# Prologue of a fused attention, mixture-of-experts and gated-MLP kernel: the third quarter of the inner weights ahead of keys and values, the fourth in halves, two tiles' transposes placed among the query-key products

## What is computed

```python
def _attn_ref(q, k, v, g_norm):                      # 8 heads of 64
    kv = np.einsum('bhsd,bhse->bhde', k, v)
    out = np.einsum('bhsd,bhde->bhse', q, kv)
    rms = np.sqrt(np.mean(out * out, axis=-1, keepdims=True) + 1e-06)
    return out / rms * g_norm
def _moe_ref(x, w_gate, wq, wk, wv, wo):             # 4 experts of width 64, top 2
    for e in range(E):
        q, k, v = x @ wq[e], x @ wk[e], x @ wv[e]
        a = causal_softmax(q @ k.T / 8)
        ye = a @ v @ wo[e]
        out += gate[e] * ye
def _moe2_ref(x, w_in, g_ln, w_sg, b_sg, w_out):     # d_ff 1024
    h = gelu(x @ w_in); u, v = split(h)
    v_s = w_sg @ layernorm(v, g_ln) + b_sg
    return x + (u * v_s) @ w_out
```

## Time and profile before

| | us |
|---|---|
| median of three runs | 814.02 |
| the profiled execution, its time | 816.52 |
| its span, first to last instruction | 814.4 |
| TensorE busy | 798.5 |
| VectorE busy | 489.7 |
| ScalarE busy | 371.3 |
| GpSimd busy | 186.3 |

### The profile page before, as it was taken

How to read it: one execution, slowest core, us unless ns; L and a number is a source line. 1 busy time by engine, 2 the same in 40 slices (tenths; PEclk the granted TensorE clock), 3 DMA queues, 4 the chain that set the end, 5 groups by cost and what they waited for, 6 DMA issues and landing times. The chain is left out here.

```text
span 814.4 us, 16834 instructions
## 1 busy us (share of the span) xinstructions
PE 798.5 (98%) x6605; PEld 720.0 (88%) x6605; DVE 489.7 (60%) x1293; ACT 371.3 (46%) x845; POOL 186.3 (23%) x239
## 2 busy tenths in 40 slices
PE   6999999999999999999999999999999999999998
PEld 5888989989899898989889898998989989898896
DVE  3878654675447855487444865468554675547740
ACT  2767423663345533556134752356323653355521
POOL 1641332013310233002330123301331013300220
PEclk9999999999999999999999999999999999999999
DMA  9956023030231205040050401404023000100001
GB/s 258 255 129 164 2 45 86 11 109 1 52 73 51 68 1 117 15 118 1 1 111 14 119 1 37 94 2 118 1 50 75 2 2 1 59 14 2 1 2 64
DMA packets 117405, 47.28 MB, mean 58 GB/s; under 512 B 94352, under 2 KB 110736, under 8 KB 117328
## 3 DMA queue, kind: packets, MB, share of 16 engines
q1 hardware_dynamic: 117328, 46.21, 22.6%
HBM read 35.19 MB, written 9.44 MB: 55 GB/s over the span
## 5 line engine op out<-in xcount | busy, mean ns | idle before, releaser
L1070 PE MATMUL w<-wsgT_s,big 128*128 128x288 f32 x768 | 107.6, 296 | 0.0
L1070 PE MATMUL t<-big,wqk_s 128*128 128x288 f32 x768 | 106.0, 296 | 1.0 <-DVE wsgT_s L950 0.9
L1070 PEld LDWEIGHTS w<-wsgT_s,big 128*128 128x128 f32 x768 | 104.0, 189 | 0.0
L1070 PEld LDWEIGHTS t<-big,wqk_s 128*128 128x128 f32 x768 | 102.5, 188 | 1.6 <-DVE wsgT_s L950 1.1
L1070 PE MATMUL w<-wout_s,big 128*128 128x512 f32 x396 | 99.1, 399 | 0.0
L610 POOL TENSOR_TENSOR yT<-squares,yT 128x256 fp32r<-128x256 f32 (+1 forms) x32 | 22.4, 699 | 316.8 <-ACT yT L740 316.8
L844 DVE CUSTOM_DVE_ANT_0 w<-w,causal 128x64 f32<-128x64 f32 (+4 forms) x160 | 75.3, 515 | 24.2 <-PE w L1101 23.1
L1070 PEld LDWEIGHTS w<-wout_s,big 128*128 128x128 f32 x396 | 72.9, 188 | 17.2 <-DVE big L887 1.6
L754 ACT ACTIVATE big<-work 128x576 fp32r<-128x576 f32 x32 | 21.9, 686 | 113.5 <-POOL work L633 94.3
L1070 PE MATMUL t<-w_s,yT 128*128 128x512 f32 x240 | 63.3, 404 | 0.0
L956 DVE TENSOR_REDUCE ss<-squares 128x8 f32<-128x512 f32 (+1 forms) x40 | 25.2, 630 | 62.6 <-ACT squares L690 62.5
(11 more groups left out here) (140 smaller groups left out, 1439.3 us busy)
## 6 DMA issues: line engine op xcount, KB each, us to landing
kin<-in_k_dram SPq DMA_DIRECT2D x8, 1024.0 KB, 6.2
vin<-in_v_dram SPq DMA_DIRECT2D x8, 1024.0 KB, 9.2
out_dram<-work SPq DMA_DIRECT2D x32, 256.0 KB, 2.1
qin<-in_q_dram SPq DMA_DIRECT2D x112, 72.0 KB, 2.4
staged_win<-in_moe_w_in_dram SPq DMA_DIRECT2D x4, 512.0 KB, 5.4
vin<-in_moe_w_sg_dram SPq DMA_DIRECT2D x4, 288.0 KB, 3.9
kin<-in_k_dram SPq DMA_DIRECT2D x8, 128.0 KB, 2.9
vin<-in_v_dram SPq DMA_DIRECT2D x8, 128.0 KB, 7.0
```

The source lines that it names most:

```text
L1070: last = nc.tensor.matmul(o, stationary(hs, c), mv(hm, c), start=c == of[0] and p == 0, stop=c == of[-1] and p == len(PASSES) - 1)
```

## The change

The prologue's list is written in another order. Quarter 2 of w_in (`win` 2 and `w2` 2) stands ahead of `kv`. The product of quarter 3 is cut in two steps, `w2c` 0 and `w2c` 1, of six matmuls each (one wide slot each). The query tiles' transposes are no longer together: tiles 3 and 4 come after x 0 and x 1. The x steps of tiles 3 and 4 leave the prologue: they are carried out in part 0 by a new step kind, `late`, which on each engine calls `body(part - 1, [j])`; one stands behind the first `qk` and `split` wv, the other behind the second `qk` and `w2e` 0. The loads follow: w_in quarter 2 ahead of k and v, g_norm ahead of q, quarter 3 between q tiles 2 and 3. Slots change with it. No arithmetic is added or taken away; the number of matmuls, copies and bytes is the same.

```diff
-    FIRST = [("woT", 0), ("woT", 1), ("win", 0), ("win", 1), ("w2", 0), ("w2", 1)] + [("kv", c) for c in range(DC)]
-    FIRST += [("qT", 0), ("qT", 1), ("qT", 2), ("o", 0), ("qT", 3), ("o", 1), ("qT", 4), ("win", 2), ("o", 2),
-              ("o", 3), ("w2", 2), ("x", 0), ("o", 4), ("win", 3), ("x", 1), ("x", 2), ("split", "wqk0"), ("split", "wqk2"), ("split", "wqk1"), ("split", "wqk3"), ("w2", 3), ("x", 3), ("x", 4)]
+    FIRST = [("woT", 0), ("woT", 1), ("win", 0), ("win", 1), ("w2", 0), ("w2", 1), ("win", 2), ("w2", 2)]
+    FIRST += [("kv", c) for c in range(DC)]
+    FIRST += [("qT", 0), ("qT", 1), ("o", 0), ("qT", 2), ("o", 1), ("o", 2), ("win", 3), ("x", 0), ("qT", 3), ("o", 3), ("x", 1),
+              ("qT", 4), ("w2c", 0), ("o", 4), ("split", "wqk0"), ("split", "wqk2"), ("x", 2), ("w2c", 1),
+              ("split", "wqk1"), ("split", "wqk3")]
+    FIRST_LATE = [("x", 3), ("x", 4)]
+    FIRST_SLOT = {("woT", 0): "t0", ("woT", 1): "t1", ("kv", 0): "t3", ("qT", 0): "t0", ("qT", 1): "t1", ("o", 0): "t2", ("qT", 2): "t0",
+                  ("o", 1): "t3", ("o", 2): "t0", ("x", 0): "t2", ("qT", 3): "t1", ("o", 3): "t1", ("x", 1): "t2", ("qT", 4): "t3",
+                  ("o", 4): "t3", ("x", 2): "t0", ("x", 3): "t2", ("x", 4): "t3"}
...
-        plan = [("qk", (0, 0))] + late(("split", "wv")) + [("qk", (EP, 0))] + late(("w2e", 0))
+        plan = [("qk", (0, 0))] + late(("split", "wv"), ("late", FIRST_LATE[0])) + [("qk", (EP, 0))] + late(("w2e", 0), ("late", FIRST_LATE[1]))
...
-            load_win((0, 1))
+            load_win((0, 1, 2))
             load_kv(0)
-            load_q(0)
-            load_win((2, 3))
             for a in range(2):
                 sp.dma_start(gnorm_c[HD * a:HD * (a + 1), :],
                              g_norm.rearrange("(p a) -> p a", a=1)).then_inc(w_loaded["gnorm"], 16)
+            load_q(0, (0, 1, 2))
+            load_win((3,))
+            load_q(0, (3, 4))
...
-                for kind, j in PLAN[part]:
+                for kind, j in PLAN[part] if among is None else among:
+                    if kind == "late":
+                        body(part - 1, [j])
+                        continue
```

More of the change, by code:

```diff
@@ L191, in ring @@
             turn[0] += 1
-        for kind, j in PLAN[part]:
+        for kind, j in PLAN[part] + (FIRST_LATE if part < 0 else []):
             if kind == "s":
@@ L450, in load_kv, with load_q @@
                                  ).then_inc(kv_loaded, 16)
-            def load_q(b):
-                sp.dma_start(qin[PAD:P, 0, :].rearrange("p (h d) -> p h d", h=H),
-                             q[b, :, 0:PAD, :].rearrange("h s d -> s h d")).then_inc(q_first[0], 16)
-                for t in range(1, NT):
+            def load_q(b, ts):
+                for t in ts:
+                    if t == 0:
+                        sp.dma_start(qin[PAD:P, 0, :].rearrange("p (h d) -> p h d", h=H),
+                                     q[b, :, 0:PAD, :].rearrange("h s d -> s h d")).then_inc(q_first[0], 16)
+                        continue
                     sp.dma_start(qin[:, t, :].rearrange("p (h d) -> p h d", h=H),
@@ L568, in _, with body @@
             before_loop = steps[0] + NT
-            def body(part):
+            def body(part, among=None):
                 done = [0]
@@ L1158, in body @@
                         finish(last, U)
-                    elif kind == "w2":
-                        pe.wait_ge(woT_hi, j // 2 + 1)
-                        pe.wait_ge(win_hi, j + 1)
+                    elif kind in ("w2", "w2c"):
+                        chunk, among_c = (j, range(EP)) if kind == "w2" else (DC - 1, [j])
+                        pe.wait_ge(woT_hi, chunk // 2 + 1)
+                        pe.wait_ge(win_hi, chunk + 1)
                         for p, (hs, hm) in enumerate(((HI, HI), (LO, HI), (HI, LO))):
                             if p == 1:
-                                u.wait_drained(pe, part, ("woT", j // 2))
+                                u.wait_drained(pe, part, ("woT", chunk // 2))
                             if p == 2:
-                                pe.wait_ge(win_lo, j + 1)
-                            for c in range(EP):
+                                pe.wait_ge(win_lo, chunk + 1)
+                            for c in among_c:
                                 x = ps[u.slot(part, ("w2", c))]
                                 for h in range(2):
-                                    last = nc.tensor.matmul(x[:, FF * h:FF * (h + 1)], woT_split[:, hs, 256 * j + P * c:256 * j + P * (c + 1)],
-                                                            win_split[j][:, hm, FF * h:FF * (h + 1)], start=j == 0 and p == 0,
-                                                            stop=j == DC - 1 and p == 2)
-                                if j == DC - 1 and p == 2:
+                                    last = nc.tensor.matmul(x[:, FF * h:FF * (h + 1)],
+                                                            woT_split[:, hs, 256 * chunk + P * c:256 * chunk + P * (c + 1)],
+                                                            win_split[chunk][:, hm, FF * h:FF * (h + 1)],
+                                                            start=chunk == 0 and p == 0, stop=chunk == DC - 1 and p == 2)
+                                if chunk == DC - 1 and p == 2:
                                     finish(last, ("w2", c))
```

5 lines of the change are left out of this document (1 added, 4 removed).

## The result

The changed kernel takes 818.37 us in the median of five runs (817.34 to 820.17), the kernel before 814.11 us beside it (five runs, 814.0 to 814.68). The medians lie 4.3 us apart. The ratio on record is 1.0046 with an interval of 1.0035 to 1.0058, which makes 3.7 us slower, 2.8 to 4.7. Forecast were 818.6 us and 4.55 us.

The account below looks back on a forecast made before the run. TensorE, busy 98% of the span, was taken as the bound, with `v` 0 as the mark. 1.94 + 0.98 + 1.1 + 0.6, less rounding 4.55 us, added to 814.02 gave 818.6 us; range 816.8 to 820.2.

Parts of the forecast that it names:

- The bound: Whole kernel: TensorE is busy 98% of the span, so a shift at `v` 0 reaches the end undiminished.
- Keys and values: Before `kv`: quarter 2's product fills TensorE's wait, the values come 1.4 us later, `kv` starts at 17.75 against 16.36.
- their 512 KB go ahead of the values on the one queue: Loads before `kv`: quarter 2's bytes delay the values by 1.4 us, or 1.83 at the stretch's rate.
- fit into the gap: TensorE before `kv`: quarter 2's 12 matmuls, 3.0 us or less, fit between 13.54 and 16.36 us.
- The chain behind `kv`: From `kv` on: cover for the o-to-x steps is lost, so the first query-key product starts at 37.0, 1.94 us later.
- The edits that were put at no cost: Prologue loads: wq and wk, and the last w_sg load waiting for query tile 4 (cover of 1.8 us), cost nothing.
- The late tiles: Query-key stretch: x 3 and x 4 add 0.98 us, plus gaps of 1.1 and 0.6 before the third and fourth products.
- The rule on ports: Tile 4's GpSimd power meets wqk2's VectorE low half: the skill's exclusive lock would add 1.5 us; forecast assumed no stretch.
- rival of stretched low halves: Beside tile 4's power: wqk2's low half starts at 36.95, first query-key product at 38.4, total 820.0 us; chance 0.12.
- faster: Behind `kv`: TensorE does not wait for the o-to-x way, total 811.6 us; chance 0.04.
- no change: After `v` 0: a later wait absorbs the shift, total 814 to 815.6 us; chance 0.06.
- No gap for late tiles: Query-key stretch: slots or VectorE are free in time, 1.7 us fall away, total 816.9 us; chance 0.14.

Follow-up runs that it names:

- e1: Kernel before with only quarter 2 of w_in (load, halves, product) moved ahead of `kv`; 815.5 against 815.58 us.
- e11: Kernel before with quarter 2 ahead of `kv`, query tiles 3 and 4 behind o 2, splits reordered, plus 11 early unused transposes; 816.76 against 815.71 us.
- e6: Changed kernel plus 11 unused transposes of the identity before TensorE's wait for the first load; 818.49 us, 2.9 us slower than the kernel before.
- before again: Kernel before, unaltered, run beside itself for a second profile; ratio 1.0004 (0.9994 to 1.0014).
- e2: Kernel before with only x 3 and x 4 moved among the query-key products, loads and slots kept; 817.93 against 815.58 us.
- e5: Changed kernel with each late x tile one step earlier, ahead of the split of wv and of `w2e` 0; 818.57 against 815.58 us for before.
- e8: Changed kernel with small unused matmuls filling TensorE's gaps before x 0, o 3, x 1 and the first query-key product; 819.87 us, 3.0 slower than before.
- e10: Kernel before with quarter 2 ahead of `kv`, query tiles 3 and 4 behind o 2, splits reordered, quarter 3's product ahead of wqk2; 817.16 against 815.71 us.
- e3: Changed kernel with x 3 and x 4 put back at the end of the prologue; 820.46 against 815.58 us for the kernel before.
- e7: Changed kernel with x 3 and x 4 back at the prologue's end and 20 unused transposes ahead of x 4; ratio to before 1.0037.

## Why the prediction held, and where its steps did not

**The bound.** Right. In the last column of the table, what follows `v` 0 has two values: 770.8 to 771.3 us in six profiles, 772.5 to 772.9 in eight. The kind of kernel doesn't decide which: the change has both. They are told apart by the granted clock from 750 to 755 us, 1.00 in the six and 0.66 to 0.81 in the eight. So a shift at `v` 0 comes out whole at the end, and beside it there is 1.7 us by chance. All five runs of before beside the change lay between 814.0 and 814.68, while its medians beside e1 to e11 were 815.6 to 815.8. The windows of the change, first and second profile (the window of the first has more idle time, since the kernel is 3 us later there):

```profile
750.00:755.00 5.00, 3.58 (x23) 0.70 0.00 2
```

```profile
750.00:755.00 5.00, 4.89 (x60) 1.00 0.00 0
```

The profiles of before and of the change both have the higher value, so they may be compared: 3.6 us of span, 3.87 at `v` 0.

**Keys and values.** The start was forecast at 17.75 and was 17.39 in the first profile and 16.25 in the second, and not for the reason given: this hit was luck. Two terms were wrong. One is "their 512 KB go ahead of the values on the one queue", priced at 1.4 us later values. The other is that the 24 products take 6.57 us and the 12 behind them "fit into the gap". The price of the bytes is near: ScalarE took quarter 2 at 8.57, 1.49 us after quarter 1 at 7.08. Yet the values landed at 5.57 + 10.4 = 16.0 us, no later than before (wait ended at 16.36). These are the issue row and the row of SyncE's queue in the change:

```profile
vin<-in_v_dram SPq DMA_DIRECT2D x1, 1024.0 KB, 10.4
```

```profile
5.57 2.60 SPq L452 DMA_DIRECT2D vin<-in_v_dram  x1
8.21 2.83 SPq L503 DMA_DIRECT2D gnorm_c<-in_g_norm_dram  x2
11.08 0.62 SPq L458 DMA_DIRECT2D qin<-in_q_dram  x1
```

What held `kv` was TensorE, which was busy without a break until then: 24 products in 7.74 us where before they took 6.57, then 12 more. In e6, where the first products were faster and nothing else ahead of `kv` differs, `kv` started at 15.90.

How much the 512 KB delay the values can be asked of all fourteen profiles, by the start of the issue plus the time to landing. With the old order of loads that gives 16.3, 17.0 and 14.9 us (before, before again, e2), 16.1 on average. With quarter 2 ahead it gives 15.7 to 16.3 in seven profiles, 16.9 in e5, and 18.1, 17.8 and 18.6 in e8, e10 and e11, 16.6 on average. So 0.5 us, not 1.4, with a spread of 2 to 3 us in each group that leaves it open whether there is any delay. The profiles in which TensorE is seen to wait for the values can't answer it alone, since behind the extra 12 products mostly the late landings show as a wait.

**The chain behind `kv`.** Right in every gap, and this is the main part of the forecast. Forecast gaps before o 0, x 0, o 3, x 1, first, third and fourth query-key product: 0.4, 1.1, 1.5, 1.3, 1.7, 1.1, 0.6. Measured: 0.34, 0.94, 1.19, 1.04, 1.54, 1.04, 0.34. Forecast length from `kv` to `v` 0 28.35 us, measured 28.04, and the engines that release TensorE are the ones named. The gaps were mostly a little too large. One reason that the rows show is the hand-off of 0.1 us: tile 1's square ends at 24.08 and VectorE's sum starts at 24.11, its power ends at 26.82 and the scaling starts at 26.85. The edits that were put at no cost show none: the wait for `wsgT_s` is 0.9 us as before.

**The late tiles.** The mechanism is right (e2, e5); the two gaps were 1.04 and 0.34 us, forecast at 1.1 and 0.6. What the prediction did not say is that they pay for themselves in part: in this order they also avoid x 4's late arrival (e3, e7), so that they cost 0.7 us and not 2.6. What e3 was expected to show, a kernel faster than the change, did not come: it was slower, by what its lower clock cost. With the gap filled (e7) the way from `kv` to `v` 0 is 0.7 us shorter than in the change, and the totals can't tell the two apart.

**The rule on ports.** The rival of stretched low halves is out: VectorE's low halves of wqk0 and wqk2 took 1.29 us for both, near the 1.2 forecast, and x 2's 0.74. (The prediction gives the price of that rival once as 1.5 us and once as 820.0 us in all; its own steps, 38.4 against 37.0, make 1.4.) But it was the order of the two engines that decided, and the prediction had it the other way round: the power did not start at 35.3 ahead of wqk2's low half; VectorE was there first, and GpSimd waited. GpSimd's timeline, tiles 2, 3 and 4, then VectorE's:

```profile
27.06 1.64 POOL L597 TENSOR_TENSOR rms_inv<-ss,neg_half 128x8 f32<-128x8 f32 x1
30.73 0.20 POOL L596 TENSOR_TENSOR ss<-ss,eps_t 128x8 f32<-128x8 f32 x1 [2.03 <-DVE ss L971]
31.01 1.64 POOL L597 TENSOR_TENSOR rms_inv<-ss,neg_half 128x8 f32<-128x8 f32 x1
34.38 0.58 POOL L596 TENSOR_TENSOR ss<-ss,eps_t 128x8 f32<-128x8 f32 x1 [1.74 <-DVE ss L971]
35.04 1.97 POOL L597 TENSOR_TENSOR rms_inv<-ss,neg_half 128x8 f32<-128x8 f32 x1
```

```profile
27.46 1.22 DVE L947 TENSOR_TENSOR wout_s<-staged_win,wout_s 128x1024 fp32r<-128x1024 f32 x1
...
34.22 1.29 DVE L952 TENSOR_TENSOR wqk_s<-staged_wqk,wqk_s 128x512 fp32r<-128x512 f32 x2
```

Tile 4's epsilon (0.58 against 0.20) and power (1.97 against 1.64) both began inside VectorE's pair, from 34.22 to 35.51, and took 0.38 and 0.33 us more than tile 3's. The Trainium skill (SBUF — State Buffer, "SBUF: two separate sides") says that whichever engine came first holds the shared ports for its whole instruction. These rows agree for VectorE coming first, as far as spans on GpSimd can be relied on, which are rough in the profile. For GpSimd coming first they don't: quarter 3's low half began at 27.46 inside tile 2's power (27.06 to 28.70) and took 1.22 us, as quarter 2's did before. The loss of 0.7 us falls on tile 4's scaling (it starts at 37.11), for which only the late x 4 waits.

**The total.** 818.6 forecast, 818.37 measured, and the two measurements of the change give 3.7 us (2.8 to 4.7) and 4.2 us (2.6 to 5.8), and the forecast shift of 4.55 lies in both intervals. That the median came within 0.3 us of the forecast is luck, since it holds 1.7 us of chance in the last part and a start of `kv` that moved by 1.1 us between two profiles. What repeats is the length from `kv` to `v` 0: 2.84 us more than before in both, against 3.15 forecast. The rivals "faster" and "no change" are excluded: `v` 0 stands at 45.43 and 44.28, above the 43.2 given as the limit, and the shift arrives at the end. "No gap for late tiles" (816.9) would put `v` 0 at 44.4 and isn't excluded by that mark, nor by the totals; it is excluded by the gaps of 1.04 and 0.34 us in both profiles.

## What to carry to other kernels

Work that fills a wait is worth the wait only if it was not covering another latency where it stood; count what TensorE would have beside each chain of small steps (here o to x: square, sum, power, scale, some 4 us, from 23.48 to 27.54 for tile 1 in the change) before moving it. Where a step moves across engines' queues, walk every queue by its own rows, since the release of a slot stands behind whatever that engine was given in between. Compare executions by marks inside the changed stretch (start of one step, length to another), since the rest of this kernel has two lengths 1.7 us apart.

## What the runs showed of the hardware that was not expected

- The first products of an execution run at less than their later rate for a time that varies: the same 24 matmuls took 6.57 and 7.35 us in the two profiles of before and 7.74 and 6.61 in those of the change. After early transposes (e6) eight took 2.08 us and the other sixteen 3.92. A single one takes 628 ns at first and 389 later, and they start some 0.43 us apart at first and 0.23 later. The last one of 628 ns or near it starts at 8.0 and 9.6 us in the two profiles of before and at 10.6 and 8.0 in those of the change. The view of the tile `wo_s` from 9 to 10 us, the change and then before (least, median and most):

```profile
L1190 PE MATMUL w<-wsgT_s,wo_s x4: 628/628/628, 8.4 to 9.7; 128*128 128x512 f32 x4
L1171 PE MATMUL w<-wsgT_s,wo_s x6: 388/392/504, 8.7 to 9.9; 128*128 128x512 f32 x6
```

  The column of the granted clock has 1.00 for both. Yet 239 ns more for 512 columns is 0.47 ns a column, and where that column has 0.50 (e3, 39 to 40 us) a query-key matmul of 288 columns takes 442 ns in place of 294, 0.51 a column. So the first products probably ran at the lower level of 1.2 GHz too (an estimate from these rows). Why the step comes at another time in each execution stays open.
- Behind gaps of 1 to 2.8 us the granted clock fell to half in some executions (e3: 0.57 from 27 to 31; e5: the same) and not in others with the same gaps (both profiles of the change). After the values' wait it fell in one profile of before and not in the other. The profiles with filled gaps had no fall (e7, e8), but neither had both of the change. What decides between like executions stays open.
- The same holds for the wait of 2.0 us in the last part, in every profile: 16 transposes behind it took 3.34 us in one and 1.97 in another. This is worth the 1.7 us between the two lengths of the rest. The rows, first of before and then of e1:

```profile
747.76 1.06 PE L1101 MATMUL w<-big 64*128 64x288 f32 x12 [2.04 <-ACT staged L718]
748.75 3.34 PE L1116 MATMUL t<-ident,staged 128*128 128x128 f32 x16
```

```profile
747.05 1.07 PE L1101 MATMUL w<-big 64*128 64x288 f32 x12 [2.06 <-ACT staged L718]
748.04 1.97 PE L1116 MATMUL t<-ident,staged 128*128 128x128 f32 x16
```
